# Slots among feed-forward products: turn, values, scores in place of scores, values, turn

## The chip, the cores and the metric

The kernel runs on one NeuronCore of a Trainium2 chip. The metric is the device time of one execution in microseconds. All inputs and outputs are float32.

## What is computed

Windowed attention with four sink keys, then two feed-forward layers on its output, 1536 tokens of 512 features:

```python
scores = scale * np.matmul(q, k.transpose(0, 1, 3, 2))      # q, k, v: 2 x 8 x 768 x 64
keep = is_sink | in_window                                  # 4 sinks, window of 128
scores = np.where(keep, scores, -1000000000.0)
a = np.exp(scores - np.max(scores, axis=-1, keepdims=True))
a = a / (np.sum(a, axis=-1, keepdims=True) + 1e-09)
attn_out = np.matmul(a, v)
...
x = (silu(x @ w_gate) * (x @ w_val)) @ w_out                # 512 -> 1536 -> 512, stage B
h = x @ w_in                                                # 512 -> 2048, stage C
out = (np.maximum(h, 0.0) + alpha * np.minimum(h, 0.0)) @ w_out2
```

## The kernel before, in words

Attention is cut into 48 units: 12 quads c (two batches of six tiles of 128 tokens), each with four head pairs g; unit u is 4c + g. One unit goes through five steps:

- scores (TensorE, `scores`, lines 1784 to 1792): both heads of the pair, against the tile's own keys, the four sink keys and the tile before. In the first tile of a batch (quads 0 and 6) there is no tile before, and scores, spread and values are half as wide.
- mask and maximum (VectorE, `take`, line 2166, 2157 in a first tile; `maximum`, line 2177), then bias, exponentials and denominators (ScalarE, `exps`, lines 2003 to 2012; a table load stands ahead of them where ScalarE last did a silu).
- reciprocal (VectorE, `invert`, line 2182) and normalisation (GpSimd, `normalise`, line 1733).
- turn (TensorE, `turn`, lines 1809 and 1812): two 128x128 transposes through the identity, a third one of the sinks' probabilities in the last unit of a quad. Then the spread (VectorE, `spread`, lines 2193 or 2197) to SBUF, each half of the window by its mask.
- values (TensorE, `values`, line 1830): eight matmuls, four in a first tile. In the last unit of a quad four sink products follow (line 1840), and x of that quad is complete. ScalarE copies it (line 2026) and rounds it to `x_hi` (line 2032), VectorE takes the rest, `x_lo` (line 2212).

Every feed-forward product is made of three float32r passes (high by high, low by high, high by low), so weights, x and hidden values are each split in a high and a low part; GpSimd splits the weights (lines 1652 and 1653). Groups of two 128-wide columns of the hidden layer go through fronts (TensorE, line 1881), silu or relu (ScalarE), the hidden product (VectorE, line 2283), its rounding (ScalarE, line 2108) and rest (VectorE, line 2300), backs (TensorE, line 1966) and evacuation (VectorE, line 2309). The other two blocks of 512 tokens follow later, in a form with seven strips in place of eight (line 1940).

The order is written out once in the list `plan`, and each engine walks that list and issues what is its own; every engine runs its own instructions in that order, and semaphores tie the engines together. An item `("slot", (u, u-1, u-2, u-3))` is one step of the software pipeline of attention: scores of unit u, reciprocal and normalisation of u-1, turn and spread of u-2, values of u-3. Units 0 to 15 (`early` is 16) go through 19 slots in the first 40 us. The other 32 units go through 35 slots: one right behind those, 34 spread evenly among 76 pieces of feed-forward work (`part_one`, six matmuls each), to about 205 us. In these late slots there is one place in PSUM for scores (two banks), one bank for the turn and one bank for x: the scores of u wait for the exponentials of u-1, the turn of u-2 for the spread of u-3 and for its own normalisation, the first values of a quad for ScalarE's copy of the last x. Behind a slot that completes a quad the plan puts `("x", c)` and then `("x_rest", c)`, so ScalarE's copy stands behind the exponentials of that slot, and VectorE's rest of x ahead of its next products and slots.

Right behind the last slots but two the last group of stage B ends, its sums are rounded by ScalarE (line 2112), VectorE takes the rest (line 2330), and the first fronts of stage C (line 1881) read them.

In a slot, before the change, TensorE does scores, values, turn, and VectorE mask, maximum, reciprocal, spread. SyncE issues all loads of keys, values and weights in an order of its own, behind waits for the scores and values of three quads before.

Of the kernel before, what the change touches and what calls it, by code (L numbers as in the profile page):

```python
# [804 lines left out]
def build_windowed(nc, qt, kt, vt, vs, pieces, alpha_t, out, n_batch, n_sink, ff_b, ff_c, scale):  # L805
# [7 lines left out]
    early = quads_t * n_pairs  # L813
# [155 lines left out]
    for n, chunk in enumerate(part_one):  # L969
        what, key = chunk  # L970
# [74 lines left out]
    turn = (backs(groups_c[3]) + fronts(groups_c[4]) + fronts(groups_c[5]) + backs(groups_c[4]) + strips(groups_c[0], 0))  # L1045
# [237 lines left out]
    with ctx:  # L1283
# [239 lines left out]
        def sum_sb(stage, n):  # L1523

            q11, q21, q12, q22 = quarters[stage]
            return {"T1": q11, "T2": q22 if stage == "B" else t2_sum, "T3": q12, "T4": q21}[T_ORDER[stage][n]]

        def slot_of_raw(r):

            job = jobs[raw_users(raws[r - n_raw]) - 1]  # L1530
            return slot_of_job.get(job, len(slot_plan) if job in late_jobs else early)
# [237 lines left out]
        def _(pe):  # L1769
# [143 lines left out]
            def strip(g, part, i):  # L1913
                m = (g, part)
                a_name, b_name, role = STRIPS[i]
                kind, n, at = CELL[a_name]
                if kind == "f":
                    pe.wait_ge(split_done, job_no["piece", piece_key(g, n, part, pair[0])])
                else:
                    pe.wait_ge(split_done, job_no["sum", (g, part, 2 * n + at)])  # L1920
                if m in (sets[0], (groups_c[0], 0)):
                    if b_name[0] == "T":
                        pe.wait_ge(tlo_done, thi_no[g[0], b_name, half_k - 1])
                    elif g[0] == "B":
                        pe.wait_ge(xlo_done, x_rests_until(quads_t * (3 if b_name == "B22" else 2) - 1))
                    else:
                        pe.wait_ge(x2lo_done, x2_no[{"B11": (1, half_k - 1), "B21": (1, n_k - 1), "B22": (2, n_k - 1)}[b_name]])
                first = i in (0, 1, 4)
                if first:
                    wait_for_bank(m, role)  # L1930
                elif i == 2:
                    pe.wait_ge(kept_done, keep_no[m])
                else:
                    pe.wait_ge(mix_done, mix_no[m, {3: 0, 5: 1, 6: 2}[i]])
                ps = strip_ps(m, role)
                w_parts = cell(operand_cell(g, part, a_name))
                b_parts = operands[b_name]
                for kk in range(half_k):
                    for a, b in PASSES:
                        last = pe.matmul(ps, w_parts[a][:, block_cols(at * half_k + kk)], b_parts[b][:, kk, :],  # L1940
                                         start=first and kk == 0 and (a, b) == (0, 0),
                                         stop=kk == half_k - 1 and (a, b) == (1, 0), skip_group_check=True)
                last.then_inc(front_done, 1)
# [33 lines left out]
            for what, n in plan:  # L1977
                if what == "front":
                    front(*n)
                elif what == "back":  # L1980
                    back(*n)
                elif what == "strip":
                    strip(*n)
                elif what == "slot":
                    if n[0] == 2:
                        keep_busy(6, bank(att_ps, 2))
                    if n[0] is not None:
                        scores(n[0])
                    if n[3] == early - 2:
                        turn(n[2])  # L1990
                        values(n[3])
                    else:
                        if n[3] is not None:
                            values(n[3])
                        if n[2] is not None:
                            turn(n[2])
# [150 lines left out]
        def _(dve):  # L2147
# [32 lines left out]
            def invert(u):  # L2180
                dve.wait_ge(dens_done, u + 1)
                dve.reciprocal(inv[:, u % 4, :], dens[:, u % 4, :]).then_inc(inv_done, 1)  # L2182
# [159 lines left out]
            for what, n in plan:  # L2342
                if what == "slot":
                    u, exped, turning, _ = n
                    if u is not None:
                        take(u)
                        maximum(u)
                    if exped is not None:
                        invert(exped)
                    if turning is not None:  # L2350
                        spread(turning)
                elif what == "x_rest":
                    rest_of_x(n)
                elif what == "hidden":
                    product(n)
                elif what == "rest":
                    rest_of_hidden(n)
                elif what == "mix":
                    mix(*n)
                elif what == "evac":  # L2360
                    evacuate(*n)
                elif what == "x2_rest":
                    rest_of_x2(*n)
                elif what == "tlo":
                    rest_of_sum(*n)
# [63 lines left out]
```

## Time and profile before

| | us |
|---|---|
| median of three runs | 639.23 (639.03 to 640.42) |
| the profiled execution | 640.56 |
| its span | 638.80 |
| TensorE busy | 622.8 |
| GpSimd busy | 451.8 |
| VectorE busy | 410.1 |
| ScalarE busy | 244.3 |

The span is what the profiler saw of the engines' work; the profiled execution's own time is 1.8 us longer. In a timeline the first column is an instruction's start, the second its duration, both in us; neighbours of a kind are merged, with their number behind the x, and what stands in brackets is the idle time of the engine before it and who ended it. Ends of matmuls are modelled (a matmul over 512 columns is shown with 0.39 us while the next starts 0.23 us behind), so distances between starts tell more than durations.

### The profile page before, as it was taken

The page shows a single profiled execution, that of the slowest core. Times are in us where ns is not written, and L with a number is a line of the kernel's source. Part 1 is how long each engine was busy: PE and PEld are TensorE (multiplying, and loading weights), DVE is VectorE, ACT ScalarE, POOL GpSimd, SP SyncE. Part 2 cuts the span into 40 slices and gives each one's busy share as a digit, 9 for nine tenths or more (in the row PEclk, how much of TensorE's full clock was granted, in tenths as well). Part 3 has the DMA queues.
Part 4 walks back from the last instruction along what each step waited for, and adds up shares of the span by engine and source line. Part 5 has one row for each costly group of instructions (what it writes and reads, how often), then busy time and mean ns, then how long its engine had stood idle before and what let it go on. Part 6 is the DMA issues. An engine that isn't in the chain of part 4 may idle for free.

```text
span 638.8 us, 9474 instructions
## 1 busy us (share of the span) xinstructions
PE 622.8 (97%) x3072; PEld 488.0 (76%) x3072; DVE 410.1 (64%) x696; ACT 244.3 (38%) x585; POOL 451.8 (71%) x600
## 2 busy tenths in 40 slices
PE   8889999999999999999999999999999999999998
PEld 5467676776776888878788878888788888888886
DVE  4954566655476876564656474799686567756474
ACT  4735644545534642121212121435544333442150
POOL 6848698796985889998989664779999887810000
PEclk9999999999999999999999999999999999999999
DMA  9343323311331011221202222000212222000004
GB/s 299 110 149 110 123 80 136 117 51 50 100 95 43 30 35 34 76 74 48 67 33 67 82 84 63 25 30 16 67 67 66 67 66 84 17 0 1 1 14 184
DMA packets 29391, 45.67 MB, mean 71 GB/s; under 512 B 2880, under 2 KB 9024, under 8 KB 29344
## 3 DMA queue, kind: packets, MB, share of 16 engines
q1 hardware_dynamic: 29200, 44.81, 21.7%
q8 instruction: 25, 0.41, 0.3%
q10 hardware_dynamic: 144, 0.26, 0.1%
q14 instruction: 22, 0.18, 0.1%
HBM read 41.92 MB, written 3.15 MB: 71 GB/s over the span
## 4 chain that ended last, share of the span: by engine, by line
PE 85%; DVE 7%; ACT 3%; issue 3%; DMA 1%; POOL 0%; SPq 0%; DVEq 0%; ACTq 0%; POOLq 0%
PE ffn_ps L1966 27%; PE att_ps L1940 22%; PE ffn_ps L1881 14%; PE att_ps L1966 7%; PE ffn_ps L1940 6%; PE att_ps L1830 3%; PE att_ps L1792 2%; PE att_ps L1809 1%; DVE scratch L2193 1%; ACT scratch L2008 1%; PE att_ps L1881 1%; DVE scratch L2309 1%; ACT L2008 1%; DMA raw_weights<-pieces 1%; PE ffn_ps L1830 1%
## 5 line engine op out<-in xcount | busy, mean ns | idle before, releaser
L1653 POOL TENSOR_TENSOR w_lo<-raw_weights,w_hi 128x512 fp32r<-128x512 f32 (+1 forms) x128 | 154.4, 1206 | 10.3
L1652 POOL CAST w_hi<-raw_weights 128x512 fp32r<-128x512 f32 (+1 forms) x128 | 79.2, 619 | 38.0 <-PE ffn_ps L1966 20.5
L2309 DVE TENSOR_TENSOR scratch<-ffn_ps,scratch 128x512 f32<-128x512 f32 x112 | 76.4, 687 | 34.9 <-PE ffn_ps L1966 34.2
L1681 POOL TENSOR_TENSOR w_lo<-part_sum,w_hi 128x256 fp32r<-128x256 f32 x80 | 61.1, 764 | 6.4
L1881 PE MATMUL ffn_ps<-x_hi,w_hi 128*128 128x512 f32 x152 | 61.8, 406 | 2.1 <-DVE x_lo L2330 1.0
L1881 PE MATMUL ffn_ps<-x_hi,w_lo 128*128 128x512 f32 x152 | 59.5, 391 | 0.0
L1881 PE MATMUL ffn_ps<-x_lo,w_hi 128*128 128x512 f32 x152 | 59.2, 390 | 0.0
L1733 POOL TENSOR_TENSOR scratch<-scratch,inv 128x264 f32<-128x264 f32 (+1 forms) x48 | 31.2, 649 | 31.8 <-DVE inv L2182 31.5
L1966 PE MATMUL ffn_ps<-h_hi,w_hi 128*128 128x512 f32 x130 | 51.6, 397 | 0.0
L1966 PE MATMUL ffn_ps<-h_hi,w_lo 128*128 128x512 f32 x130 | 50.7, 390 | 0.0
L1966 PE MATMUL ffn_ps<-h_lo,w_hi 128*128 128x512 f32 x130 | 50.6, 389 | 0.0
L2098 ACT ACTIVATE value_sb<-att_ps 128x512 f32<-128x512 f32 x14 | 8.4, 600 | 100.3 <-PE att_ps L1940 100.3
L1940 PE MATMUL att_ps<-t_hi,w_hi 128*128 128x512 f32 x112 | 44.5, 398 | 1.3 <-DVE gate_sb L2232 0.8
L1940 PE MATMUL att_ps<-t_hi,w_lo 128*128 128x512 f32 x112 | 44.0, 392 | 0.0
L1940 PE MATMUL att_ps<-t_lo,w_hi 128*128 128x512 f32 x112 | 43.7, 391 | 0.0
L1940 PE MATMUL att_ps<-x_hi,w_hi 128*128 128x512 f32 x108 | 42.7, 395 | 0.0
L1940 PE MATMUL att_ps<-x_hi,w_lo 128*128 128x512 f32 x108 | 42.5, 393 | 0.0
L1940 PE MATMUL att_ps<-x_lo,w_hi 128*128 128x512 f32 x108 | 42.1, 390 | 0.0
L2003 ACT ACTIVATE bias<-top 128x2 f32<-128x2 f32 x48 | 9.8, 203 | 75.5 <-DVE top L2177 75.0
L1680 POOL CAST w_hi<-part_sum 128x256 fp32r<-128x256 f32 x80 | 34.7, 434 | 5.1
L2166 DVE COPY_PREDICATED att_ps<-take_prev,att_ps 128x256 f32<-128x256 int32 x34 | 14.4, 425 | 35.8 <-PE att_ps L1792 22.3
L2087 ACT ACTIVATE gate_sb<-gate_sb,minus_alpha 128x512 f32<-128x512 f32 x48 | 34.8, 725 | 1.6
(207 smaller groups left out, 1574.9 us busy)
## 6 DMA issues: line engine op xcount, KB each, us to landing
raw_weights<-pieces SPq DMA_DIRECT2D x122, 256.0 KB, 2.7
k_sb<-kt SPq DMA_DIRECT2D x12, 264.0 KB, 3.4
v_sb<-vt SPq DMA_DIRECT2D x12, 256.0 KB, 2.7
out<-scratch SPq DMA_DIRECT2D x12, 256.0 KB, 2.0
q_sb<-qt SPq DMA_DIRECT2D x11, 256.0 KB, 3.5
scratch<-vs SPq DMA_DIRECT2D x1, 384.0 KB, 5.5
q_sb<-qt ACTq DMA_DIRECT2D x1, 256.0 KB, 2.8
alpha<-alpha_t SPq DMA_DIRECT2D x1, 8.0 KB, 6.6
```

What stands on the lines that cost most here:

```text
L1652: chain(pool.tensor_copy(hi, raw[:, r % n_raw, at]))
L1653: last = pool.tensor_tensor(lo, raw[:, r % n_raw, at], hi.bitcast(F32), ALU.subtract)
L1680: chain(pool.tensor_copy(hi, s))
L1681: pool.tensor_tensor(lo, s, hi.bitcast(F32), ALU.subtract).then_inc(split_done, 1)
L1733: pool.tensor_tensor(rows, rows, inv[:, u % 4, :].unsqueeze(2).to_broadcast([P, 2, cols - at]), ALU.mult).then_inc(norm_done, 1)
L1830: last = pe.matmul(x[d, g, :], v_sb[:, ring, g, d], pt_sb[:, u % 2, m, h, :], start=g == 0 and m == 0, stop=not has_prev(c), skip_group_ch ...
L1881: last = pe.matmul(ps, w_parts[a][:, block_cols(kk)], x_parts(kk)[b], start=kk == 0 and (a, b) == (0, 0), stop=kk == n_k - 1 and (a, b) == ...
L1940: last = pe.matmul(ps, w_parts[a][:, block_cols(at * half_k + kk)], b_parts[b][:, kk, :], start=first and kk == 0 and (a, b) == (0, 0), st ...
L1966: last = pe.matmul(ps, lhs, rhs, start=f == 0 and (a, b) == (0, 0), stop=f == F - 1 and (a, b) == (1, 0))
L2087: act.activation(gate_of(h), gate_of(h), ACT.Copy, scale=minus_alpha[:, col:col + 1]).then_inc(relu_done, 1)
L2166: last = dve.copy_predicated(own_keys, take_prev[:, :].bitcast(mybir.dt.int32).unsqueeze(1).to_broadcast([P, 2, P]), s[:, :, 0:P])
L2309: ins = dve.tensor_tensor(total, back_ps(key), total, ALU.add)
```

## The change

In the late slots TensorE does the turn first, then the values, then the scores; VectorE does reciprocal and spread first, then mask and maximum. ScalarE, GpSimd and SyncE keep their order. The early slots keep theirs on all engines.

```diff
+        def beside(units):
+
+            return any(u is not None for u in units) and min(u for u in units if u is not None) >= early
+
...
+                elif what == "slot" and beside(n):
+                    if n[2] is not None:
+                        turn(n[2])
+                    if n[3] is not None:
+                        values(n[3])
+                    if n[0] is not None:
+                        scores(n[0])
                 elif what == "slot":
                     if n[0] == 2:
                         keep_busy(6, bank(att_ps, 2))
...
             for what, n in plan:
                 if what == "slot":
                     u, exped, turning, _ = n
+                    if beside(n):
+                        if exped is not None:
+                            invert(exped)
+                        if turning is not None:
+                            spread(turning)
+                        if u is not None:
+                            take(u)
+                            maximum(u)
+                        continue
                     if u is not None:
                         take(u)
                         maximum(u)
```

## Rows read from the trace of the kernel before

**Rows 1.** The page, busy us (share of the span) and instructions of TensorE

```profile
PE 622.8 (97%) x3072; PEld 488.0 (76%) x3072; DVE 410.1 (64%) x696; ACT 244.3 (38%) x585; POOL 451.8 (71%) x600
```

**Rows 2.** TensorE's waits from 40 to 210 us: total, times, longest

```profile
PE att_ps L1792 <- ACT scratch L2008: 1.6, 2, 1.1
PE att_ps L1784 <- ACT scratch L2008: 1.1, 1, 1.1
...
PE att_ps L1786 <- ACT scratch L2008: 0.6, 2, 0.4
...
PE ffn_ps L1881 <- DVE x_lo L2330: 1.0, 1, 1.0
```

**Rows 3.** The waits of all engines in the same stretch, VectorE's for `x_hi`

```profile
DVE x_lo L2212 <- ACT x_hi L2032: 16.0, 8, 3.1
```

**Rows 4.** Timeline of TensorE, a plain slot between two pieces of fronts

```profile
134.94 0.39 PE L1881 MATMUL ffn_ps<-x_hi,w_lo 128*128 128x512 f32 x1
135.26 0.71 PE L1792 MATMUL att_ps<-k_sb,q_sb 64*128 64x260 f32 x4
135.90 0.66 PE L1830 MATMUL att_ps<-scratch,v_sb 128*64 128x128 f32 x8
136.48 0.44 PE L1809 MATMUL att_ps<-ident,scratch 128*128 128x128 f32 x2
...
136.99 0.39 PE L1881 MATMUL ffn_ps<-x_lo,w_hi 128*128 128x512 f32 x1
```

**Rows 5.** Timeline of TensorE, a turn behind two fills (early slots)

```profile
36.84 0.73 PE L1973 MATMUL att_ps<-h_hi 128*128 128x512 f32 x2
37.40 0.38 PE L1809 MATMUL att_ps<-ident,scratch 128*128 128x128 f32 x2
```

**Rows 6.** Timeline of TensorE, the late slot that holds scores alone

```profile
45.91 0.50 PE L1786 MATMUL att_ps<-k_sb,q_sb 64*128 64x128 f32 x4
...
46.57 0.50 PE L1881 MATMUL ffn_ps<-x_hi,w_hi 128*128 128x512 f32 x1
46.90 0.39 PE L1881 MATMUL ffn_ps<-x_lo,w_hi 128*128 128x512 f32 x1
```

**Rows 7.** Timeline of TensorE, sink products ahead of scores, and ahead of a turn

```profile
39.75 0.66 PE L1840 MATMUL ffn_ps<-pts,v_sink 96*128 96x128 f32 x4
40.34 0.50 PE L1786 MATMUL att_ps<-k_sb,q_sb 64*128 64x128 f32 x4
...
146.66 0.66 PE L1840 MATMUL att_ps<-pts,v_sink 96*128 96x128 f32 x4
147.16 0.40 PE L1809 MATMUL att_ps<-ident,scratch 128*128 128x128 f32 x2
```

**Rows 8.** Timelines of ScalarE, VectorE and TensorE, behind the quad completed at 147

```profile
149.74 0.58 ACT L2026 ACTIVATE scratch<-att_ps 128x512 f32<-128x512 f32 x1
...
151.02 0.69 DVE L2212 TENSOR_TENSOR x_lo<-scratch,x_hi 128x512 fp32r<-128x512 f32 x1 [2.72 <-ACT x_hi L2032]
...
153.62 0.42 DVE L2166 COPY_PREDICATED att_ps<-take_prev,att_ps 128x256 f32<-128x256 int32 x1
...
154.43 0.15 DVE L2182 RECIPROCAL inv<-dens 128x2 f32<-128x2 f32 x1
...
155.09 0.68 DVE L2283 TENSOR_TENSOR gate_sb<-ffn_ps,gate_sb 128x512 f32<-128x512 f32 x1
...
155.79 0.71 PE L1792 MATMUL att_ps<-k_sb,q_sb 64*128 64x260 f32 x4 [1.11 <-ACT scratch L2008]
```

**Rows 9.** Timelines of VectorE and TensorE, behind the quad completed at 90

```profile
92.41 1.11 DVE L2212 TENSOR_TENSOR x_lo<-x_sb,x_hi 128x256 fp32r<-128x256 f32 x1 [1.64 <-ACT x_hi L2032]
93.63 0.77 DVE L2157 COPY_PREDICATED att_ps<-first_out,masked_score 128x256 f32<-128x256 int32 x1
...
97.42 0.71 PE L1792 MATMUL att_ps<-k_sb,q_sb 64*128 64x260 f32 x4 [0.43 <-ACT scratch L2008]
```

**Rows 10.** Timelines of ScalarE and TensorE, the turn from stage B to stage C

```profile
193.60 0.63 ACT L2112 ACTIVATE x_hi<-scratch 128x512 fp32r<-128x512 f32 x1
...
198.58 0.50 PE L1881 MATMUL ffn_ps<-x_hi,w_hi 128*128 128x512 f32 x1 [0.97 <-DVE x_lo L2330]
```

## Prediction

> **What bounds the kernel now.** I read the page first: TensorE is busy 622.8 of 638.8 us at the full granted clock [rows 1], so the time is TensorE's own work plus about 16 us in which it stands. The waits of the stretch in which slots lie among feed-forward products (40 to 210 us) say where: the scores wait for the exponentials 3.3 us in five places, the fronts of C for `x_lo` 1.0 us [rows 2]. The same view, over all engines, shows what the rest of x hangs on: VectorE waits 16.0 us in eight places for ScalarE's `x_hi` [rows 3]. So an attention unit is a chain scores, mask, maximum, exponentials, and ScalarE's copy of a finished x (line 2026) is queued behind those exponentials. The timelines of single slots give the lengths. What matters is where the scores stand in the slot, and what else hangs on the exponentials that follow.
>
> **Part 1, the order on TensorE.** Nothing is removed or added: 32 slots of the 34 among products (the first holds scores alone, the last values alone) change the order scores, values, turn to turn, values, scores. A plain slot runs from the last product before it to the second after it in 136.99 - 134.94 = 2.05 us: 0.32 to the scores, 0.64 to the values, 0.58 to the turn, 0.51 to the second product [rows 4]. The trace shows no turn right behind a product, but one behind a 128x512 fill: two fills take 0.73 with modelled ends 0.39 after their starts, so the second began at 37.18 and the turn 0.22 to 0.23 later, the same distance as between two products, and its pair took 0.38 where it takes 0.44 behind the values [rows 5, 4]: no gap, the second transpose 0.11 behind the first. Scores (in their narrow form, two pairs of 128 and 132 columns) with a product behind them: 0.66 to it, 0.33 more to the second [rows 6]; for the wide form I keep the 0.64 of its row. Values to scores: 0.20 from the last product's start, as in every change of shape; sink products to scores 0.59 against 0.50 to a turn [rows 7]. New plain slot: 0.23 + 0.11 + 0.20 + 0.58 + 0.64 + 0.33 = 2.09, so +0.05 (2.10 with three decimals). New slot with sink products: 0.59 more, 2.68, against 0.32 + 0.64 + 0.58 + 0.50 + 0.48 = 2.52: +0.16. Sum 26 x 0.05 + 6 x 0.16 = **+2.3 us**. Bounds: 0, if the scores' tail costs no more than the turn's; +7 if the turn pays 0.15 behind a product as it does behind the values (0.09 in the distance, 0.06 in the pair).
>
> The gaps of 0.09 at a change of tile shape are what the Trainium skill says in TensorEngine Tiling (Array Packing), Key Properties: changing the tiling mode drains the engine. But TensorE: Matmul & The Clock Gate, The mechanism, has a weight load overlap running matmuls only where the row group differs; by that the turn behind a product would pay it too, 4.7 us in all. The fill's row [rows 5] speaks against it; see the rivals.
>
> **Part 2, how much later the scores are.** Old place 0.32 behind the last product. New: 0.23 + 0.11 + 0.20 + 0.58 = 1.12 in a plain slot (0.80 later), 0.59 later where only four value matmuls stand (0.37 in place of 0.58), 1.71 where the sink products stand (1.39 later), 0.22 later in the one slot with no values. If the next slot's scores are as much later, this costs nothing: the chain and its deadline move together. It costs where they move unequally, and these are the slots with sink products, one per quad.
>
> **Part 3, VectorE's order.** Reciprocal and spread stand ahead of mask and maximum. Where VectorE is in time they fit while TensorE does values and scores: the turn's last transpose starts 0.78 ahead of the scores, which take 0.64 more. Where it comes late, mask and maximum start later by what reciprocal and spread hold the engine: from 154.43 to the next start at 155.09, 0.66 [rows 8]. A plain slot gives 0.80, so on its own this is nothing; I count the 0.14 over as nothing too. The reciprocal's wait for the denominators now stands at the head of the slot, with spread, mask and maximum queued behind it; the denominators of the slot before are ready by then. GpSimd's normalisation gets its factor about 1.5 us earlier; TensorE waits for GpSimd nowhere in this stretch [rows 2], so this gains nothing, and it keeps the turn, which is now wanted 1.3 us earlier, from waiting. If that cover were gone, in the slots behind GpSimd's pair sums, the turn would wait 0.1 to 0.4, inside a wait that the scores have anyway. SyncE's loads of keys wait for scores that are 0.6 to 1.4 later and are used slots later: nothing.
>
> **Part 4, the chain behind the sink products.** Take the slot with the sink products at 146.66. The exponentials of its scores are followed on ScalarE by the copy of x (149.74) and its rounding; VectorE takes the rest of x, a hidden product, its rest, the mask (153.62), and the next scores start at 155.79, where TensorE has stood 1.11 us [rows 8, 2]. x itself was complete at 147.3 by the sink products' row [rows 7]; the copy waited only for the exponentials, and it will again. Everything from there to the rest of the hidden product moves by 1.39, and then the spread stands ahead of the mask: + 0.66. The scores start 2.05 later; TensorE arrives 0.16 + 0.05 + 0.80 = 1.0 later. Wait: + 1.05 (a part of it shows before the values, since x's only bank is read by that copy). Behind quad 4 the pattern is the same, with 1.1 before the scores of line 1784 [rows 2]. Two quads: **+2.1**.
>
> Four more quads have the chain with slack. In the first, at 92.41, the rest of x waits 1.64 for `x_hi`; 1.39 later, at 93.80, and with the shorter spread of that quad (0.39) ahead, the mask goes from 93.63 to between 94.8 and 95.25, + 1.4, against 0.8 that TensorE is later (four values): + 0.6 on the 0.43 at 97.42 [rows 9]. In the last of the four the mask moves by 1.06 against 1.01 and no slack: + 0.1. The two between, by the same steps, + 0.4 and + 0.5. Together **+1.6**, bounds 0 and 4.2 (as the first two).
>
> **Part 5, the first fronts of C.** In the last quad the mask is 1.39 + 0.66 later; ScalarE's rounding for C at 193.60 stands behind the exponentials, so it comes 2.05 later, and VectorE's rests, evacuation and spread follow one another from there, with some of the gaps between them closed: the front at 198.58, which waits for the last rest, starts about 1.4 later [rows 10], of which 0.26 is the slots' own length: **+1.1**, bounds 0 and 1.8.
>
> **Part 6, a gain.** The second late slot has no values, so its scores are 0.22 later and the next ones 0.80: 0.58 more room, which removes the 0.4 before them, the longest of line 1786 [rows 2], with the restart **-0.5**.
>
> **Sum** 2.3 + 2.1 + 1.6 + 1.1 - 0.5 = +6.6 us. The profiled execution (640.56, span 638.80) would become 647.2; it is 1.3 above the median of the runs, so for the median 639.23 + 6.6 = **645.8 us**.
>
> **The rivals.**
> (a) Only TensorE's order counts: ScalarE or VectorE make up the lateness, since other work of theirs slides under it. 2.3 - 0.5 = +1.8, 641.0 us. For it: both are far from full. Against: the rest of x waits for `x_hi` in every quad [rows 3, 9]. Chance 0.20.
> (b) Not slower: the later scores find their bank free. The 3.3 us before the scores go, and with the spread early the 1.0 before C's fronts too [rows 2]: 2.3 - 3.3 - 1.0 = -2.0, 637.2 us; with the first alone -1.0, 638.2 us. It decides if the exponentials of one slot end less than 1.12 behind the next slot's last product, so if VectorE stands ready when the scores land. Against: in the two largest waits it stands behind the hidden product and its rest when they land, and the spread ahead of the mask makes that longer. Chance 0.10.
> (c) The turn behind a product pays 0.15 in 32 slots: +4.7 more, 650.5 us. This is the result that the page's rule on weight loads gives. Against: the fill's row. Chance 0.04.
> (d) The lateness is passed on whole: the four quads with slack cost 1.05 each (+2.6 more), and turns that wait for normalisation 0.5: +9.7, 648.9 us. Chance 0.08.
> The change does what it says: all units of the late slots are 16 or more, and no slot mixes early and late ones.
>
> **How the numbers follow.** Forecast 0.58, (a) 0.20, (b) 0.10, (c) 0.04, (d) 0.08. The range leaves out (b), (c) and the lower third of (a): 640.7 to 649.6. A measurement here tells 0.2% (1.3 us) from no change. Faster: 0.06, the larger half of (b). Same: 0.08, the rest of (b) and the low end of (a). Slower: 0.86.
>
> **What would show it.** Right: a turn 0.23 behind the product, scores 1.12 behind (1.71 behind sink products); the idle time before the values and scores near 73 to 81 and 150 to 158 doubled to some 2.2 us together; the copy of x on line 2026 about 1.4 later behind its exponentials; longer waits of the scores near 97, 115 and 135; the front of C that stood at 198.58 with over 2 us of wait. Wrong: idle before the scores that shrinks (b), or slots that are longer with no more waits (a, c). The prediction falls if VectorE or ScalarE start x's rest no later relative to the slot.

## The result, and the profile after

The changed kernel takes 647.3 us (median of 4 runs, 646.37 to 648.21), the kernel before in the same comparison 639.62 (4 runs, 639.03 to 640.42): ratio 1.012, 95% interval 1.0107 to 1.0133, so +7.7 us. Its profiled execution took 646.37 us with a span of 644.6, against 640.56 and 638.8: +5.8. A later set of runs of the same kernel gave 650.86 (5 runs, 647.92 to 651.95), ratio 1.016 [1.014, 1.0181]; its profiled execution has a span of 646.2. The two profiles of the changed kernel are called its first and its second here, and what differs between them is explained below.

The page and TensorE's waits of the changed kernel from 40 to 215 us (total, times, longest), to be read against [rows 1, 2]. Lines of TensorE and GpSimd stand 4 further down than before, lines of ScalarE and VectorE 11 further:

```profile
PE 626.8 (97%) x3072; PEld 491.8 (76%) x3072; DVE 409.0 (63%) x696; ACT 244.2 (38%) x585; POOL 450.5 (70%) x600
```

```profile
PE att_ps L1834 <- issue: 2.2, 2, 1.1
PE ffn_ps L1885 <- issue: 1.9, 1, 1.9
PE att_ps L1796 <- ACT scratch L2019: 1.4, 3, 0.8
PE att_ps L1788 <- ACT scratch L2019: 0.8, 1, 0.8
PE ffn_ps L1885 <- DVE x_lo L2230: 0.6, 1, 0.6
PE ffn_ps L1885 <- DVE x_lo L2341: 0.3, 1, 0.3
PE att_ps L1813 <- POOL scratch L1737: 0.2, 1, 0.2
```

Three of these lines matter. The values (L1834) stand in two slots, where they stood nowhere before; the first front of C waits 1.9 instead of 0.5; and the turn (L1813) now waits for GpSimd. "Issue" is what the view puts down where it shows no releaser; the timeline names it: the slots are those behind quads 4 and 8, and the values start when ScalarE's copy of x (L2037) has read its bank. TensorE and ScalarE of the changed kernel, behind the quad completed at 149; start, duration, operation, in brackets the idle time before it:

```profile
153.11 0.38 PE L1813 MATMUL att_ps<-ident,scratch 128*128 128x128 f32 x2
...
153.79 0.20 ACT L2023 ACTIVATE dens<-sums 128x2 f32<-128x2 f32 x1
153.90 0.58 ACT L2037 ACTIVATE scratch<-att_ps 128x512 f32<-128x512 f32 x1
154.51 0.63 ACT L2043 ACTIVATE x_hi<-scratch 128x512 fp32r<-128x512 f32 x1
...
154.58 0.66 PE L1834 MATMUL att_ps<-scratch,v_sb 128*64 128x128 f32 x8 [1.09 <-issue]
...
155.17 0.71 PE L1796 MATMUL att_ps<-k_sb,q_sb 64*128 64x260 f32 x4
155.18 0.69 DVE L2223 TENSOR_TENSOR x_lo<-scratch,x_hi 128x512 fp32r<-128x512 f32 x1 [3.83 <-ACT x_hi L2043]
```

Ahead of the rest of x VectorE stood idle 2.72 us before [rows 8] and stands 3.83 here. Over all 34 slots among products, each measured from the last product before it to the second one after it and two product distances (0.229) subtracted, the slots cost 57.6 us before and 63.9 after: +6.3. The thirteen slots without sink products that wait in neither kernel cost 0.044 to 0.054 more, and the six with sink products 0.170 to 0.177 more. The rest of the 6.3 is waits that grew or shrank.

The attention slots do not carry the whole difference. Between 200 and 210 us the clock fell. Busy time of each engine in stretches of the changed kernel, with the granted clock after ACT and POOL (PEclk), the DMA share and GB/s:

```profile
200.00:205.00 5.00, 2.88 (x14) 1.67 (x10) 4.64 (x8) 2.35 (x7) 1.24 (x3) 0.78 0.17 52
205.00:210.00 5.00, 5.00 (x26) 3.83 (x27) 1.86 (x4) 1.89 (x3) 1.91 (x2) 0.87 0.02 3
```

In the kernel before, the same stretches have 1.00, as this one has from 190 to 200. The products lie up to 0.43 us apart there in place of 0.23, 1.1 us in all; but the second front of C, which stood 1.0 us for `x_lo` before, stands only 0.3, since TensorE comes to it later. So the lower clock costs 0.65 us net. The second profile shows this from the other side: its clock stays at 1.00, and that front waits as before:

```profile
PE ffn_ps L1885 <- DVE x_lo L2341: 1.0, 1, 1.0
...
PE att_ps L1944 <- DVE gate_sb L2243: 0.9, 2, 0.6
```

The second line is of the strips of stage C. The kernel before stands 0.8 us there, the changed kernel 0.2 in its first profile and 0.9 in its second. From the products just ahead of the last slot to the last product six of the fourteen profiles take 431.6 to 431.9 us (the changed kernel's first among them), eight take 432.6 to 432.7 (the kernel before, the changed kernel's second). The same kernel has both, so that microsecond belongs to the execution and not to the order of the slots. So the first profile is 6.3 us in the slots, 0.65 for the clock and 1.0 less at the strips, some 5.9 against the 5.8 measured. The second is 7.5 in the slots and nothing elsewhere, against 7.4 measured, and near the +7.7 of the medians.

### The profile page after: what moved, and what is told of

Same layout as the page of the kernel before. It is cut to its first block, busy times and chain, and to the rows that moved or that the text cites. A ratio compares the mean times of both kernels' runs of the same rounds, so it can differ in the third digit from the quotient of the medians.

```text
span 644.6 us, 9474 instructions
## 1 busy us (share of the span) xinstructions
PE 626.8 (97%) x3072; PEld 491.8 (76%) x3072; DVE 409.0 (63%) x696; ACT 244.2 (38%) x585; POOL 450.5 (70%) x600
## 4 chain that ended last, share of the span: by engine, by line
PE 84%; DVE 7%; ACT 4%; issue 2%; DMA 1%; POOL 1%; SPq 0%; DVEq 0%; ACTq 0%; POOLq 0%
PE ffn_ps L1970 26%; PE att_ps L1944 22%; PE ffn_ps L1885 14%; PE att_ps L1970 7%; PE ffn_ps L1944 6%; PE att_ps L1834 2%; PE att_ps L1796 2%; DVE scratch L2204 2%; DMA raw_weights<-pieces 1%; PE att_ps L1813 1%; ACT scratch L2019 1%; DVE scratch L2320 1%; PE att_ps L1885 1%; PE ffn_ps L1834 1%; PE att_ps L1844 1%
## 5 line engine op out<-in xcount | busy, mean ns | idle before, releaser
L1885 PEld LDWEIGHTS ffn_ps<-x_hi,w_hi 128*128 128x128 f32 x152 | 28.8, 189 | 15.1 <-issue 7.6
```

The costliest lines, as they stand in the source:

```text
L1885: last = pe.matmul(ps, w_parts[a][:, block_cols(kk)], x_parts(kk)[b], start=kk == 0 and (a, b) == (0, 0), stop=kk == n_k - 1 and (a, b) == ...
```

## Experiments

The prediction's theory: the loss is the order's own price on TensorE (+2.3) and lateness of the exponentials, behind which ScalarE's copy of a finished x is queued. Rival at the start: the order alone. A third cause came up on the way (late weight loads). The kernel before ran beside every set, with medians of 639.62 to 640.21. Three edits are combined below, with the order of before and the changed one: "x ahead" puts ScalarE's copy and rounding of a finished x ahead of the slot's exponentials, "loads later" issues SyncE's key, query and value loads two slots later, and "copy ahead" moves the copy alone. Times are medians in us; the columns come from different sets.

| order of the late slots | as it is | copy ahead | x ahead | loads later | x ahead, loads later |
|---|---|---|---|---|---|
| before | 639.6 to 640.2 | 639.39 | 638.43 | not run | 638.17 |
| changed | 647.3 / 650.86 | 645.69 | 640.26 | 645.51 | 637.97 |

**e1_x_ahead: take the queue away in the changed kernel.**

```diff
+            ahead = set()
+            for at, (what, n) in enumerate(plan):
                 if what == "slot" and n[0] is not None:
+                    if n[0] >= early and plan[at + 1][0] == "x":
+                        c = plan[at + 1][1]
+                        ahead.add(c)
+                        round_x(c)
+                        round_late_x(c)
                     exps(n[0])
...
```

> The changed kernel, but ScalarE does the copy and the rounding of a finished x (lines 2026 and 2032 of before) ahead of the exponentials of the same late slot; all else as changed. Theory (the late scores cost through what is queued behind their exponentials): the waits before the values behind quads 4 and 8 (1.1 us each) vanish, the waits before the scores there shrink below the 1.1 us of before, C's first fronts wait no longer than before and TensorE's clock does not fall there; what remains is the order on TensorE, +2.3, less some waits: +0.5 to +2.5 us against before, 640.1 to 642.1. Rival 1 (the cost lies in each slot's own length or in the spread ahead of the mask): not below +5 us, over 644.6. Rival 2 (the exponentials themselves now come too late, since 1.2 us of rounding stands ahead of them): the scores' waits grow and it is as slow as the changed kernel, +7 us or more.

640.26 us (12 runs, 638.88 to 642.77), ratio to before 1.0006 [0.9993, 1.0018], as the theory expected. One queue position on ScalarE takes 7 us off the changed kernel. The slots' sum fell from 63.9 to 57.2. TensorE's waits, same stretch and columns:

```profile
PE ffn_ps L1885 <- DVE x_lo L2350: 1.0, 1, 1.0
PE att_ps L1813 <- POOL scratch L1737: 0.9, 2, 0.6
...
PE ffn_ps L1834 <- DVE scratch L2213: 0.3, 1, 0.3
```

No scores wait any more, the 2.2 before the values are gone (a 0.3 for VectorE's spread is left), and so is the 1.9 before C. What is left is the turn.

**e6_before_x_ahead: the same edit in the kernel before.** It tells whether the queue is a fault of the change or an old one.

> The kernel before, with ScalarE's copy and rounding of a finished x ahead of the exponentials of the same late slot; TensorE and VectorE as before. Theory: the waits of the scores behind quads 4 and 8 (1.1 us each) come from x's rest lying late in VectorE's queue and shrink by 0.7 each, those near 97 and 115 too; against it the exponentials of the quad's last slot are up to 1.2 us later, since x is finished 2.0 us behind the last product there and the maximum at 2.1: -2.5 to 0 us against before. Rival (both cancel): within 0.3 us of before.

638.43 us (11 runs, 637.75 to 641.88), 0.9983 [0.9971, 0.9994]: an old fault, but a cheap one, 1.4 us by the medians (639.83 beside it) and 0.6 in the slots of its profile, against 7. The waits of the scores at 78 and 155 (1.18 us each) go. In their place the scores one slot earlier stand 0.72 and 1.0 us, held by exponentials that now come behind copy and rounding; those near 97 stand 0.72 in place of 0.50.

**e4_quad_end_as_before: keep the old order only in the slots that complete a quad.** By part 4 it is their 1.39 us that hurts; all others keep the new order.

```diff
+            if units[3] is not None and units[3] % n_pairs == n_pairs - 1:
+                return False
             return any(u is not None for u in units) and min(u for u in units if u is not None) >= early
```

> The changed kernel, but the seven late slots that complete a quad keep the order of before on TensorE and VectorE; the other 28 have the new one. Theory: the scores in those slots are not 1.39 us later, so x's copy and rest come as before; left are 26 slots of +0.05 (+1.3), the spread ahead of the mask (+0.66 against 0.80 given) and the gain of 0.5 at the second late slot: +0.3 to +2 us against before, 639.9 to 641.6, with the clock full at C's first fronts. Rival (lateness of each plain slot adds up): +5 us or more, since four of five slots are still changed.

642.69 us (5 runs, 641.78 to 643.16), 1.0036 [1.0024, 1.0048]: 4.6 us of the loss are in these few slots, but the time is 1.1 us above the range expected (639.9 to 641.6). TensorE's waits tell which term was missing:

```profile
PE att_ps L1815 <- POOL scratch L1739: 1.3, 3, 0.8
...
PE att_ps L1790 <- ACT scratch L2021: 0.8, 1, 0.8
PE att_ps L1798 <- ACT scratch L2021: 0.8, 1, 0.8
```

The slots with the next scores behind quads 4 and 8 stand 1.03 and 1.0 us, little less than the 1.18 of before. The first line is the surprise: the turn waits for GpSimd's normalisation.

**e2_tensore_alone and e3_vectore_alone: each half of the change by itself.** e2 takes VectorE's new order out, e3 TensorE's:

```diff
-                    if beside(n):
-                        if exped is not None:
-                            invert(exped)
-                        if turning is not None:
-                            spread(turning)
...
-                        continue
```

```diff
-                elif what == "slot" and beside(n):
-                    if n[2] is not None:
-                        turn(n[2])
-                    if n[3] is not None:
-                        values(n[3])
-                    if n[0] is not None:
-                        scores(n[0])
```

> Only TensorE's new order; VectorE does mask, maximum, reciprocal, spread as before. Theory: the chain behind a completed quad loses the 0.66 us of the spread ahead of the mask, but reciprocal and normalisation come after the maximum, so the turn, now first in its slot, waits for them where VectorE is late (behind quads 4 and 8 by about 1 us): between -1 and +1 us of the changed kernel, +6.7 to +8.7 against before, with waits of the turn for normalisation of 1 us and more in all, where the changed kernel has 0.2. Rival (VectorE's order is the cost): +2 to +4 us against before.

> Only VectorE's new order; TensorE does scores, values, turn as before. The spread then waits for the turn at the slot's end while the scores stand ready, so the mask starts about 1.9 us later behind its scores, and the scores' place is not later. Theory: a slot's scores wait for the exponentials in nearly every late slot, about 1 us each, +20 to +35 us against before, over 659 us, on the waits of the scores. Rival (VectorE's order costs by its own only behind completed quads): +1 to +5 us.

TensorE alone: 651.03 us (5 runs, 649.94 to 654.58), 1.0178 [1.0157, 1.0199]: +10.8, 2.1 above the top of its range. VectorE alone: 662.11 (4 runs, 661.76 to 665.18), 1.0351 [1.0332, 1.037], as expected. TensorE's waits in e2 (first two lines), then in e3:

```profile
PE att_ps L1813 <- POOL scratch L1737: 6.3, 9, 1.4
PE att_ps L1834 <- issue: 2.6, 3, 1.1
```

```profile
PE att_ps L1796 <- ACT scratch L2012: 9.8, 7, 2.3
PE att_ps L1788 <- ACT scratch L2012: 3.9, 2, 2.3
PE att_ps L1790 <- ACT scratch L2012: 2.8, 3, 1.3
```

In e3 the spread cannot start before a turn that TensorE still does last, and the mask is queued behind it: 16.5 us of waits. In e2 the reciprocal stays behind mask and maximum while the turn that needs its product comes 1.3 us earlier: 6.3 us in nine places. So VectorE's new order is what keeps the turn from waiting, as part 3 says of the early reciprocal, but the cover is thin. Two halves that lose 11 and 22 us lose 8 together: parts of an order are not priced one by one.

**c_changed_again: the changed kernel once more**, beside e6, e7 and e8 on the same chip.

> The changed kernel once more, beside the next ones on the same chip: +7.1 to +7.9 us against before, and a granted clock below 1.00 behind the wait of C's first front in the profiled execution, with products some 0.43 us apart there.

650.86 us, 3.6 above the first set and +11.0 where +7.1 to +7.9 was expected. Its five runs fall in two groups: 647.92 and 648.40 us at a mean granted clock of 1.0, and 650.86, 651.66 and 651.95 at 0.992, 0.995 and 0.992. The profiled one is of the first group, so the lowered clock that was expected in it is not there. In it the turn at 123 us waits 1.27 us where it waited 0.46 in the first profile. GpSimd of the first profile, with the turn that waits for it, and then GpSimd of this one:

```profile
119.26 0.61 POOL L1656 CAST w_hi<-raw_weights 128x512 fp32r<-128x512 f32 x1 [1.64 <-DMA raw_weights<-pieces]
...
121.21 0.63 POOL L1737 TENSOR_TENSOR scratch<-scratch,inv 128x264 f32<-128x264 f32 x1
...
121.98 0.41 PE L1813 MATMUL att_ps<-ident,scratch 128*128 128x128 f32 x2 [0.24 <-POOL scratch L1737]
```

```profile
120.46 0.61 POOL L1656 CAST w_hi<-raw_weights 128x512 fp32r<-128x512 f32 x1 [2.41 <-DMA raw_weights<-pieces]
121.15 1.28 POOL L1657 TENSOR_TENSOR w_lo<-raw_weights,w_hi 128x512 fp32r<-128x512 f32 x1
122.39 0.63 POOL L1737 TENSOR_TENSOR scratch<-scratch,inv 128x264 f32<-128x264 f32 x1
```

The normalisation has its factor but stands on GpSimd behind a cast and a rest of weights, and the cast waits for their transfer. Why the transfer is late, SyncE's queue says: its waits from 100 to 126 us, in the changed kernel's first profile,

```profile
SPq L1568 <- POOL w_lo L1657: 8.3, 4, 3.3
SPq L1562 <- PE att_ps L1834: 5.9, 1, 5.9
SPq L1553 <- PE att_ps L1796: 4.2, 1, 4.2
```

against 2.9 us for the last of these lines in the kernel before. The key load (L1553) overwrites keys that scores still read; the scores are 0.8 to 1.4 us later, the load waits with them, and the weight loads (L1568) are queued behind it; e10 tests this. In all, GpSimd waits for weights 1.3 us in one place before, 6.1 in four places after, 7.0 here.

**e7_fill_before_c: is it the clock?** Eight pairs of matmuls with the identity fill TensorE's stand before C's first front; nothing is taken from their output.

```diff
+                    if n[1] == n_units - 1:
+                        pe.wait_ge(exp_done, 2 * n_units)
+                        for _ in range(8):
+                            pe.matmul(att_ps[:, 0:P], ident[:, :], ident[:, :], start=True, stop=True,
+                                      skip_group_check=True)
```

> The changed kernel, but TensorE does eight small products (identity by identity, 128 columns, some 1.7 us in all, into the bank of the last scores) behind the values of the slot after which it stands for C's first front. They compute nothing that is used. Theory (TensorE's clock falls because it has stood there 1.8 us, and the fall costs by itself): the fills lie in the wait, the clock stays at 1.00, the products behind are 0.23 apart, and the time is 0.9 to 1.6 us below the changed kernel. Rival (the clock falls for what TensorE did before, or the products there are slow for another reason): no change of time, or 0.2 us more.

646.98 us (5 runs, 645.93 to 648.93), ratio 1.0117 [1.0102, 1.0132], at a granted clock of 0.999 to 1.0 in every run. The group above 650 us is gone, which is what the fill was to do: the median is 3.9 us below the 650.86 beside it. Against the two runs of the changed kernel at full clock (647.92, 648.40) no gain is shown, since the fill's own runs spread over 3 us; its profiled one took 648.58. That the upper group goes with the lowered clock is shown by its 0.992 to 0.995 and by the fill. With the fill C's first front starts right behind it, and its products follow at 0.23 us from the second one on:

```profile
202.13 2.05 PE L1998 MATMUL att_ps<-ident 128*128 128x128 f32 x16
204.02 0.47 PE L1885 MATMUL ffn_ps<-x_hi,w_hi 128*128 128x512 f32 x1
```

**e8_copy_ahead: how much lateness costs how much.** Only the copy of x (0.58 us) goes ahead of the exponentials, the rounding stays behind them.

> The changed kernel, but ScalarE does only the copy of a finished x (line 2026 of before) ahead of the exponentials of the same late slot; the rounding (line 2032) stays behind them. Theory (the binding chain goes through the rounding and VectorE's rest of x, not through the values' bank): the 1.1 us waits before the values behind quads 4 and 8 vanish, but the scores of the next slot wait as much more, up to 2 us instead of 1; the copy's 0.6 us is off the chain only where the exponentials do not come 0.6 later for it. Time -2 to 0 us against the changed kernel. Rival (the wait before the values is a cost of its own): -2.2 us for the two waits and more, -2.5 us or below.

645.69 us (6 runs, 643.07 to 648.43), 1.0095 [1.007, 1.0119]. That is 5.2 us below the changed kernel beside it, and 2.9 between the two profiled executions, both at a clock of 0.999 or 1.0 (spans 643.3 and 646.2): more than the 0 to 2 of the theory, and by the time alone the rival's range. The waits say otherwise. Behind quads 4 and 8 the wait before the values is gone, and the slot that follows stands 1.58 us, 0.65 of it before the turn and 0.9 before the scores. TensorE's waits in e8 (the 1.4 is the turn near 122):

```profile
PE att_ps L1813 <- POOL scratch L1737: 2.4, 3, 1.4
...
PE att_ps L1796 <- ACT scratch L2019: 1.1, 2, 0.8
```

Each of the two places gains 0.6, the copy's own length, and not the 1.1 of a whole wait. The same 0.5 to 0.7 comes near 98 and 137 and before C's first front, which the expectation had not counted; these five places make up the 2.9, and smaller changes cancel.

**e10_loads_later: is it SyncE's queue?** In the changed kernel:

```diff
-                if n_pairs * c - 5 <= n and c < n_quads:
+                if n_pairs * c - 3 <= n and c < n_quads:
...
-                if n_pairs * c - 8 <= n and n % n_pairs == 0 and c < n_quads and c > RING + 1:
+                if n_pairs * c - 6 <= n and n % n_pairs == 2 and c < n_quads and c > RING + 1:
```

> The changed kernel with one edit: SyncE issues the loads of keys and queries, and those of values, two slots later, so that the weight loads queued behind them on SyncE do not stand behind a key load that still waits for scores. Theory A (the turn's waits near 122 come from GpSimd's normalisation, which stands behind weight casts that wait for late loads): GpSimd's waits for the raw weights fall from 6 to 7 us to under 2, the turn's wait near 122 (0.48 in the changed kernel, 1.2 in its second run) goes, and the kernel is 0.4 to 1.5 us faster than the changed kernel: 646 to 648. Theory B (the normalisation is late for its own work on GpSimd, not for loads): the turn's wait stays and the time is that of the changed kernel, 647.3 to 650.9.

645.51 us (6 runs, 645.41 to 649.69), 1.0101 [1.0083, 1.012]. GpSimd's waits for weights are gone from its list altogether, the key load waits 1.4 us for the scores from 100 to 126 us where it waited 4.2, and the turn near 122 us no longer waits. Its one wait for GpSimd that is left (0.2 us, at 184) is there without any late load. GpSimd of e10, in the same place as in the two fences above: no idle time ahead of the casts, and the normalisation at 120.58.

```profile
118.65 0.61 POOL L1656 CAST w_hi<-raw_weights 128x512 fp32r<-128x512 f32 x1
119.34 1.28 POOL L1657 TENSOR_TENSOR w_lo<-raw_weights,w_hi 128x512 fp32r<-128x512 f32 x1
120.58 0.63 POOL L1737 TENSOR_TENSOR scratch<-scratch,inv 128x264 f32<-128x264 f32 x1
```

Five of the six runs lie within 645.41 to 645.93 at a clock of 1.0. The changed kernel at that clock took 646.77 in its first set and 647.92 and 648.40 in its second, so late loads cost 1.3 to 2.9 us by the times. In the profiled slots it is 1.4 against the second profile, 1.27 of it the turn near 122. The sixth run is at 0.994 and took 649.69. It is the profiled one; its stretches show the clock (columns as above, the clock is the third number from the end):

```profile
200.00:203.00 3.00, 1.12 (x12) 0.74 (x11) 3.00 (x6) 2.17 (x7) 1.10 (x2) 1.00 0.29 85
203.00:205.00 2.00, 1.80 (x6) 0.92 (x5) 1.90 (x4) 0.74 (x2) 0.74 (x2) 0.71 0.01 4
205.00:207.00 2.00, 1.59 (x4) 1.31 (x5) 0.35 (x1) 0.00 (x0) 0.00 (x0) 0.50 0.00 0
207.00:209.00 2.00, 2.00 (x9) 1.25 (x9) 0.00 (x0) 0.58 (x1) 0.53 (x1) 0.50 0.00 0
```

From C's first front to the end this execution takes 2.4 us more than the changed kernel's second profile, whose clock is 1.00: that is the fall's price, and not all of the 4.2 that the run is above the other five.

**e11_before_x_ahead_loads_later and e12_x_ahead_loads_later: both edits, in either order.** With nothing late, what is the order itself worth?

> The kernel before with two edits: ScalarE copies and rounds the finished x ahead of the slot's exponentials (as in e6_before_x_ahead, 638.43) and SyncE issues key, query and value loads two slots later. In the order of before nothing waits for the normalisation, so theory A gives no more than e6_before_x_ahead has: 637.8 to 638.8, against 639.2 to 640.2 for the kernel before. If late weights cost time in another place too, it is below 637.8; if a key load becomes late, it is above 639.

> The changed kernel with the two edits of e1_x_ahead and e10_loads_later together. e1_x_ahead took 640.26, with 0.9 us of waits of the turn for the normalisation and 10.4 us of GpSimd's waits for raw weights. Theory A: both go, 639.3 to 640.0. Theory B: 640.0 to 640.6, with the turn's waits still there. Either way it stays above the kernel before with x ahead (638.43), because the turn ahead of the values still costs 0.05 in each slot: 26 x 0.05 = 1.3 us.

e11: 638.17 us (9 runs, 637.95 to 638.7), 0.9975 [0.9966, 0.9985], as expected; not to be told from e6 (638.43). e12: 637.97 (9 runs, 637.19 to 640.02), 0.9971 [0.996, 0.9983]: 2.3 us below e1 (1.9 when each is set against the kernel before beside it; 1.4 in the profiled slots), which confirms the late loads, and 1.3 below the range expected. That expectation had e12 above the old order by the order's price. It was wrong, and the two profiles side by side show why. TensorE's waits from 40 to 215 us, all of them, in e11:

```profile
PE att_ps L1792 <- ACT scratch L2008: 1.8, 3, 0.9
PE ffn_ps L1881 <- DVE x_lo L2339: 1.0, 1, 1.0
PE ffn_ps L1881 <- DVE x_lo L2228: 0.6, 1, 0.6
PE ffn_ps L1881 <- issue: 0.5, 1, 0.5
PE att_ps L1786 <- ACT scratch L2008: 0.4, 1, 0.4
```

and in e12:

```profile
PE ffn_ps L1885 <- DVE x_lo L2350: 1.0, 1, 1.0
PE ffn_ps L1885 <- DVE x_lo L2239: 0.6, 1, 0.6
```

Slot by slot, e12 pays the order's price (0.047 to 0.054 in the 21 plain slots where neither waits, 0.169 to 0.176 in the six with sink products; 2.4 us in sum over all 32) and saves what e11 still stands: 0.5 at 54 us, 0.7 at 74, 0.1 at 97, 0.9 at 150 and 0.66 before C's first front. The slots cost 56.4 us in e11 and 55.9 in e12, the spans are 637.0 and 636.2. Behind quad 8 the table load ahead of the exponentials starts at 148.26 in both, 3.96 us behind the last product before the slot in e11 and 4.06 in e12, although the scores are 1.4 later in e12: in the old order ScalarE still waits for x, which is complete only behind the scores. And TensorE comes for the bank of the scores 0.8 us later. e12, e11 and e6 are all faster than both kernels of the case; among the three the intervals overlap.

**e9_before_copy_ahead: why the copy alone helps only the changed order.** (The copy is float32 to float32, as its line below shows, and not to bf16.)

> The kernel before with only the copy of the finished x to bf16 ahead of the slot's exponentials on ScalarE, and its rounding behind them as before. With both ahead it was 638.43 (0.9983 of before), where the scores of three slots still waited 0.72, 0.72 and 1.0 us for exponentials that come 1.3 us later. Theory A (what costs there is the exponentials' lateness, what gains is the scores not waiting behind the sink products): with only the copy ahead (0.58 us) those three waits shrink or go, and the kernel is 1.2 to 2.5 us below before: 637.2 to 638.6. Theory B (the rounding behind the exponentials is as late as the copy was): the sink products' own wait returns, and it is that of before, 639.2 to 640.2.

639.39 us (11 runs, 638.96 to 640.36), 0.9995 [0.9987, 1.0004]: theory B's range, above theory A's. The waits at the ends of quads 4 and 8 are those of before (1.10 us before the scores at 155). ScalarE of e9 behind quad 8:

```profile
146.71 0.60 ACT L2026 ACTIVATE scratch<-att_ps 128x512 f32<-128x512 f32 x1 [2.22 <-PE att_ps L1840]
...
147.47 1.28 ACT L2008 ACT_TABLE_LOAD   x1
...
149.73 0.61 ACT L2032 ACTIVATE x_hi<-scratch 128x512 fp32r<-128x512 f32 x1
```

In the old order x is complete only at 146.7, when the table load for the exponentials is due. In the kernel before that load starts 2.06 us behind the slot's first scores (145.44 and 147.50), here 2.69 (144.78 and 147.47): the copy pushes the exponentials by its own length, the rounding ends 5.56 us behind those scores instead of 5.55, and the next scores stand as long as before. In the changed order x is complete before the scores (149.62 in e8, with ScalarE idle 0.93 us ahead of it and 1.08 after it), and the copy is free.

## Why the prediction was right where it was, and where not

It forecast 645.8 us in a range of 640.7 to 649.6, slower with chance 0.86; measured 647.3. Its terms against the slots of the two profiles of the changed kernel, each less the same slot of the kernel before (us):

| term | forecast | first profile | second profile |
|---|---|---|---|
| order on TensorE (part 1) | +2.3 | +2.4 | +2.4 |
| quads 4 and 8 (part 4) | +2.1 | +2.0 | +2.1 |
| the other four quads (part 4) | +1.6 | +0.5 | +0.5 |
| C's first front (part 5) | +1.1 | +1.2 | +1.2 |
| second late slot (part 6) | -0.5 | -0.5 | -0.5 |
| turns that wait (part 3) | 0 | +0.8 | +1.8 |
| all slots | +6.6 | +6.3 | +7.5 |

Where the column of a profile does not add up, it is by rounding.

**Part 1, the order's price (+2.3).** Right, and the best supported term. The turn starts 0.228 to 0.233 behind the product in 26 of 32 slots and waits in the other six; in e12, where nothing waits, it is 0.230 to 0.235 in all 32, so the 0.15 of rival (c) is not paid. Against e11, e12's plain slots cost 0.051 more on the mean against 0.05 forecast, slots with sink products 0.174 against 0.16. As a net effect of the order it is too much, however: e12 against e11 shows that the same order also takes back about 2.9 us of waits. It was counted as a cost with one gain (part 6) beside it, because the other gains need a finished x to be out of ScalarE's way.

**Part 4, quads 4 and 8 (+2.1).** Right in mechanism and size: 1.18 us in one place before, 1.15 before the values and 1.04 in the next slot after, for each of the two; +2.0. That it is the queue on ScalarE is shown by e1, where these waits vanish, and scaled by e8.

**Part 4, the other four quads (+1.6).** Three times too large. Beyond the order's price their slots changed by +0.25, -0.29, +0.45 and +0.05 against +0.6, +0.4, +0.5 and +0.1: only the last two are as worked out, and the +0.25 is the turn's wait, with the scores' wait as before. The step that put 0.4 on the second quad had the wrong sign: that quad has no sink products, the scores of the slot that completes it move by 0.59 us and not by 1.39, and the scores near 115 that stood 0.3 before stand no more. The total was close by luck: turns that wait, counted as nothing, made up 0.8 us of the 1.1 in the first profile and more than all of it in the second.

**Part 5, C's first fronts (+1.1).** Right in place and size: the first front starts 1.2 us later than its slot's price explains, in both profiles, and at a clock of 1.00 the second front waits as before. What the step did not have is what can follow a stand of 1.9 us: the granted clock. In the first profile the next products come 0.32 to 0.43 us apart instead of 0.23 until 206.2, 0.65 us net; in e10's profile it is 2.4 us.

**Part 3, "SyncE: nothing".** This is the step that failed. It asked when the keys are used (slots later, true) and not what is queued behind the load: the weight loads, then GpSimd's casts, then the normalisation, then a turn that the change itself moved to the head of the slot. Its price in the slots is 0.5 us in the first profile (the turn near 122) and 1.4 in the second (against e10), and again 1.4 between e1 and e12. "TensorE waits for GpSimd nowhere, so this gains nothing" was read from the right view [rows 2], but a cover that is thick enough for a turn at 1.5 us is not for a turn at 0.23. Nor does the turn wait inside a wait of the scores, as the part has it: near 122 and 184 the scores did not wait before. The 0.3 at 184 stays in e10, so late loads are not its cause; what is, no run here shows.

**Part 6 (-0.5).** Right: the slot at 53 us costs 0.49 less.

**The size of the difference.** The forecast is added to a profiled execution (640.56) that the prediction takes to be 1.3 above the median. It is one of those with the extra microsecond at C's strips, and the changed kernel's first profile is not. So the +5.8 between these two is not what to hold against +6.6; the +7.4 between two profiles of the same kind is.

**Rivals.** (a), only the order's price, falls: 647.3 is 6.3 us above its 641.0, and e1, which has the price without most of the waits, is at 640.26. (b), not slower, falls for this change, but its mechanism is real and is what e12 shows once x is ahead. (c) falls by the turn's 0.23. (d), lateness passed on whole with turns that wait 0.5, was the nearest rival in time and partly in mechanism: turns do wait, the four quads do not pay in full.

**What stays open.** Why the clock falls in some executions and not in others with the same stand of 1.9 us: e10 has it in one of six, the second set of the changed kernel in three of five. Why an execution has the extra microsecond at C's strips or not. And why late loads come later in one execution than in another: the turn's wait at 122 (0.46 and 1.27) is 0.8 of the 1.2 us by which the slots of the two profiles differ. The first and second sets, e1 against e12 and the changed kernel against e10 were also not run side by side; the kernel before, which was beside each, moved by no more than 0.6 us.

## What to carry to other kernels

When a step is moved, follow every in-order queue it passes two links further than the engine that executes it: here the scores moved, a load that waits for them moved, the loads behind that one moved, and the wait came up on another engine. And price a new order with its queues put in order as well: the same order of TensorE was 8 us slower than the old one, and level with it (637.97 and 638.17) when ScalarE handed on the finished x before the exponentials and SyncE issued its waiting loads later.

## What the runs showed of the hardware

A stand of 1.9 us of TensorE is followed in some executions by a stretch at the lower of its two clock levels: granted 0.50 (1.2 GHz) from 205 to 209 us in e10, products 0.43 us apart instead of 0.23, 2.4 us in that execution; it was 1.00 (2.4 GHz) up to 203 us, and TensorE had been busy 1.12 us of the 3 before. In the changed kernel's second profile the same stand is followed by a clock of 1.00 throughout. Sixteen small matmuls that use nothing but the identity, in that stand, kept the clock at 0.999 to 1.0 in all five runs. The Trainium skill, TensorE: Matmul & The Clock Gate, HAM oscillation — how this bites in real kernels, has TensorE come back throttled from each wait of its example. Here the lower level after a wait is the same, but only in some executions of one kernel, and in the first profile the mean over 205 to 210 us was 0.87 already; the measurement decides.

A turn of 128x128 transposes directly behind 128x512 products pays no gap, 0.230 to 0.235 us from the last product in all 32 slots of e12, while scores or values of 64 rows or columns directly behind such a product start 0.32 us behind it, 0.09 more.
